# Level scores of a chunked gated attention on TensorE: four 64x64 places and one visit a level in place of two visits with copied queries

## The reference

```
f = sigmoid(f_logit)
for t in range(768):
    state = f[t][:, None] * state + outer(k[t], v[t])
    y[t] = q[t] @ state
```

## Time and profile before

| | us |
|---|---|
| median of three runs | 1084.7 |
| the profiled execution | 1084.7 |
| its span | 1082.9 |
| PE busy | 1013.7 (94%) |
| VectorE busy | 539.7 (50%) |
| ScalarE busy | 454.3 (42%) |
| GpSimd busy | 449.7 (42%) |
| chain of work that ended last: PE's share | 85% |

### The profile page before, as it was taken

One profiled execution on the slowest core, in us unless ns is written; L12 is line 12 of the kernel. 1 busy time (PEld: TensorE's weight loads), 2 busy tenths in 40 slices (PEclk: granted clock), 3 DMA queues, 4 the chain that ended last, 5 costly groups with the idle time before them and its releaser, 6 DMA issues.

```text
span 1082.9 us, 19234 instructions
## 1 busy us (share of the span) xinstructions
PE 1013.7 (94%) x7816; PEld 828.0 (76%) x7816; DVE 539.7 (50%) x743; ACT 454.3 (42%) x840; POOL 449.7 (42%) x368
## 2 busy tenths in 40 slices
PE   1484999999999999999999999999999999999997
PEld 1473778778777877877788888888888888888886
DVE  3965894885688388659736532222223222232221
ACT  6456647544753665375336532222122221222221
POOL 1856982764475366537526522212121221212121
PEclk9666999999999999999999999999999999999999
DMA  9323005202400600130043100010010010000000
GB/s 358 153 86 130 1 2 166 79 2 75 159 13 2 215 31 1 44 115 30 2 176 131 45 30 30 1 59 1 1 59 1 1 59 1 30 1 1 30 1 29
DMA packets 17367, 63.52 MB, mean 59 GB/s; under 512 B 1920, under 2 KB 2176, under 8 KB 16512
## 3 DMA queue, kind: packets, MB, share of 16 engines
q1 hardware_dynamic: 17280, 62.30, 15.9%
HBM read 52.85 MB, written 9.44 MB: 58 GB/s over the span
## 4 chain that ended last, share of the span: by engine, by line
PE 85%; issue 5%; ACT 4%; DVE 3%; POOL 2%; DMA 0%; POOLq 0%; ACTq 0%; SPq 0%; DVEq 0%
PE acc L447 11%; PE acc L448 10%; PE acc L449 10%; PE bank L474 7%; PE bank L473 7%; PE bank L475 7%; PE bank L346 6%; PE hid L433 6%; PE hid L434 5%; PE hid L435 5%; ACT scores L527 2%; PE hid L474 2%; PE hid L475 2%; PE hid L473 2%; PE bank L378 2%
## 5 line engine op out<-in xcount | busy, mean ns | idle before, releaser
L929 POOL TENSOR_TENSOR g_lo<-prod,g_hi 128x512 fp32r<-128x512 f32 x72 | 93.1, 1293 | 347.4 <-ACT g_hi L652 347.4
L922 POOL TENSOR_TENSOR g_lo<-act_tmp,g_hi 128x512 fp32r<-128x512 f32 x96 | 140.0, 1459 | 182.0 <-ACT g_hi L613 182.0
L827 DVE TENSOR_TENSOR sig<-sig,bank 128x512 f32<-128x512 f32 x72 | 49.5, 688 | 275.4 <-ACT sig L646 275.4
L740 DVE COPY_PREDICATED scores<-mask,bank 64x512 f32<-64x512 int32 x144 | 134.5, 934 | 32.7 <-PE bank L346 31.0
L652 ACT CAST g_hi<-prod 128x512 fp32r<-128x512 f32 x72 | 44.7, 621 | 247.8 <-PE acc L449 247.8
L433 PE MATMUL hid<-x_hi,win_hi 128*128 128x512 f32 x288 | 119.1, 414 | 16.1 <-DVE act_tmp L815 16.1
L882 POOL TENSOR_TENSOR keys<-keys,gates 128x512 f32<-128x512 f32 x82 | 108.0, 1317 | 57.5 <-PE bank L346 46.1
L613 ACT CAST g_hi<-act_tmp 128x512 fp32r<-128x512 f32 x96 | 59.5, 620 | 166.0 <-DVE act_tmp L815 166.0
L346 PEld LDWEIGHTS bank<-right_q,keys 128*64 128x64 f32 x2304 | 79.9, 148 | 62.4 <-issue 59.8
L346 PE MATMUL bank<-right_q,keys 128*64 128x64 f32 x2304 | 89.6, 236 | 39.6 <-ACT right_q L548 36.3
L447 PE MATMUL acc<-g_hi,wout_hi 128*128 128x512 f32 x288 | 116.9, 406 | 4.7 <-POOL g_lo L922 4.7
(11 more groups left out here) (79 smaller groups left out, 1858.7 us busy)
## 6 DMA issues: line engine op xcount, KB each, us to landing
gates<-in_f_dram SPq DMA_DIRECT2D x12, 512.0 KB, 5.4
queries<-in_q_dram SPq DMA_DIRECT2D x12, 512.0 KB, 4.9
keys<-in_k_dram SPq DMA_DIRECT2D x12, 512.0 KB, 4.8
values<-in_v_tok_dram SPq DMA_DIRECT2D x6, 1024.0 KB, 8.2
q_tok<-in_q_tok_dram SPq DMA_DIRECT2D x12, 384.0 KB, 8.1
k_tok<-in_k_tok_dram SPq DMA_DIRECT2D x12, 384.0 KB, 8.3
x_dram<-x_out SPq DMA_DIRECT2D x6, 768.0 KB, 3.2
x_raw<-x_dram SPq DMA_DIRECT2D x6, 768.0 KB, 5.5
```

Source lines behind the costliest of these rows:

```text
L740: last = dve.copy_predicated(o, level_mask(li, half), t[rows(half), :].rearrange("p (x b r) -> p x b r", x=BP, r=m))
L922: pool.tensor_tensor(g_lo[:, c % RING, :], act_tmp[:, 2 + c % 2, :], g_hi[:, c % RING, :].bitcast(F32), ALU.subtract).then_inc(g_lo_done, 1)
```

## The change

- `right_q`, its clearing and `copy_right` are gone. `level` reads the queries themselves. Each product is of one head: 64 partitions (a head's) by 64 columns of keys against 32 right queries, in the place of the array that head and half give: four places of 64x64. The two heads write into two banks.
- A level is one visit of TensorE over all 16 pairs and both heads (64 products; the last level 32), and signals `filled` by two at its end. `scale_q` and `scale_k` of both groups wait for that end.
- `take_level(a, li, e)` is by head: VectorE takes head 0 in the level's half chunk, behind the two scalings, and head 1 in the next one, for the first five levels. ScalarE takes both heads of the last two, whose entries need no mask.
- Plans are tuples: `USUAL` for units 2 to 5, with levels at half chunks (1, 4, 7, 10, 13, 16, 18); `SECOND` for unit 1, levels at (6, 9, 12, 14, 16, 18, 20), placing of the diagonal at 0, 2, 3, 4 and sigmoids at 3, 4; `FIRST` for unit 0. Unit 1 is no longer late, and its `own` and `sum_own` stand in the prologue.
- In unit 0 VectorE places the diagonals with two broadcast multiplications; ScalarE's first activation is a dummy sigmoid ahead of the data; the loads come group by group; w_in's pieces are split at every second half chunk from 4.

```diff
-H_STEP = (1, 3, 5, 7, 8, 9, 10, 12, 13, 14, 15, 17, 18, 19)
+USUAL = Plan(own=(-9, -8), diag=(-8, -7), place=(-6, -5, -4, -3), sigmoid=(-2, -1), gated=(-1, 0),
+             level=(1, 4, 7, 10, 13, 16, 18), y=(20, 20, 21, 21), y_out=(20, 21, 21, 22),
+             tk=(22, 22, 23, 23), tk_out=(23, 23, 24, 24), kv=24, decay=21, state=25, state_place=26)
+SECOND = Plan(own=(-9, -8), diag=(-8, -7), place=(0, 2, 3, 4), sigmoid=(3, 4), gated=(4, 5),
+              level=(6, 9, 12, 14, 16, 18, 20), y=(22, 22, 23, 23), y_out=(22, 23, 23, 24),
+              tk=(24, 24, 25, 25), tk_out=(25, 25, 26, 26), kv=26, decay=23, state=27, state_place=28)
+FIRST = USUAL._replace(diag=(-3, -2), sigmoid=(-3, -2), gated=(-3, -2))
...
+            for x in range(BP):
+                for half in range(2 if li < NL - 1 else 1):
+                    for e in range(2):
+                        t = slice(half * HALF, (half + 1) * HALF)
+                        if li < NL - 1:
+                            o = of(a, 2 * li + e)[rows(half), x * HALF // 2:(x + 1) * HALF // 2]
+                            q_right = queries[rows(e), x, t].rearrange("p (b s r) -> p b s r", s=2, r=m)[:, :, 1, :]
...
+                        last = pe.matmul(o, keys[rows(e), x, t], q_right, start=True, stop=True)
+            last.then_inc(filled, 2)
...
         def scale_q(a, s):
-            dve.wait_ge(q_copied, a * STEPS + s + 1)
+            dve.wait_ge(filled, fill(a, 2 * li + 2))
...
+            for li in levels_at(a, h - 1):
+                if li < NL - 2:
+                    take_level(a, li, 1)
+            for li in levels_at(a, h):
+                for g in range(2):
+                    scale_q(a, 2 * li + g)
+                if li < NL - 2:
+                    take_level(a, li, 0)
...
+        def place_diag(a, g):
+            d = diag[:, g * BP:(g + 1) * BP].rearrange("p (x a) -> p x a", a=1).broadcast_to([P, BP, P])
+            i = eye[:, :].rearrange("p (a t) -> p a t", a=1).broadcast_to([P, BP, P])
+            dve.tensor_tensor(o, i, d, ALU.mult).then_inc(diag_placed, 2)
```

More of the change, by code:

```diff
@@ L1 @@
+from collections import namedtuple
 from contextlib import ExitStack
@@ L32 @@
 PIECE = 2 * DM
+STEPS = 2 * NL
+MASKED = 2 * (NL - 2)
 Y0 = STEPS
@@ L338, in level @@
             if li:
-                pe.wait_ge(k_scaled, a * STEPS + s - 1)
+                pe.wait_ge(k_scaled, a * STEPS + 2 * li)
             else:
[L341 to L351, removed]
@@ L406, in attention @@
         def attention(a, h):
-            for s in ladder(h):
-                level(a, s)
+            for li in levels_at(a, h):
+                level(a, li)
             for b in range(B):
-                if H_Y[b] == h:
+                if PLANS[a].y[b] == h:
                     outputs(a, b)
@@ L521, in place_diag @@
                 act.wait_ge(diag_done, 2 * a + b // 2 + 1)
-            if b == 0 and a > 0:
+            if b == 0:
                 act.wait_ge(filled, fill(a - 1, TK0))
@@ L528, in place_diag, with take_level @@
             last.then_inc(diag_placed, 1)
[L530 to L539, removed]
-                if li < NL - 1:
[L541 to L545, removed]
-                else:
-                    i = i[:, :, HALF:P].rearrange("p x (s t) -> p x s t", s=2)
-                last = act.copy(o, i)
-            last.then_inc(q_copied, 1)
+        def take_level(a, li, e):
+            act.wait_ge(filled, fill(a, 2 * li + 2))
+            act.wait_ge(dve_took, a * DVE_A_UNIT + MASKED)
+            t = bank[fill(a, 2 * li + e) % 3]
+            for half in range(2):
+                if li < NL - 1:
+                    r = slice(half * HALF, half * HALF + HALF // 2)
+                    o = scores[r, :, e, (2 * half + 1) * HALF // 2:(half + 1) * HALF]
+                    last = act.copy(o, t[r, :].rearrange("p (x i) -> p x i", x=BP))
+                else:
+                    o = scores[rows(0), half::2, e, HALF:P]
+                    last = act.copy(o, t[rows(half), :].rearrange("p (x i) -> p x i", x=BP // 2))
+            last.then_inc(act_took, 1)
         def take_keys(a, b):
@@ L572, in attention @@
             for b in range(B):
-                if H_PLACE[b] == h:
+                if a > 0 and PLANS[a].place[b] == h:
                     place_diag(a, b)
             for g in range(2):
-                if H_SIGMOID[g] == h:
+                if PLANS[a].sigmoid[g] == h:
                     sigmoid(a, g)
-            for s in ladder(h + 1):
-                copy_right(a, s)
+            for li in levels_at(a, h):
+                if li >= NL - 2:
+                    for e in range(2):
+                        take_level(a, li, e)
             for b in range(B):
-                if H_Y_OUT[b] == h:
+                if PLANS[a].y_out[b] == h:
                     split_y(a, b)
@@ L723, in scale_q, with take_level @@
             dve.tensor_tensor(qr, qr, left.broadcast_to([P, BP // 2 * P // (2 * m), m]), ALU.mult).then_inc(q_scaled, 1)
[L725 to L728, removed]
+        def take_level(a, li, e):
+            dve.wait_ge(filled, fill(a, 2 * li + 2))
             if li:
[L730 to L733, removed]
+                dve.wait_ge(dve_took, a * DVE_A_UNIT + 2 * li + e - 1)
+            else:
+                dve.wait_ge(diag_placed, B * (a + 1))
+            if a == 0 and li == 0:
                 dve.wait_ge(mask_in, 16)
[L735 to L747, removed]
+            m = LEVELS[li]
+            t = bank[fill(a, 2 * li + e) % 3]
+            for half in range(2):
+                o = scores[rows(half), :, e, half * HALF:(half + 1) * HALF]
+                o = o.rearrange("p x (b s r) -> p x b s r", s=2, r=m)[:, :, :, 1, :]
+                last = dve.copy_predicated(o, level_mask(li, half),
+                                           t[rows(half), :].rearrange("p (x b r) -> p x b r", x=BP, r=m))
             last.then_inc(dve_took, 1)
@@ L873, in scale_k @@
             m = LEVELS[li]
-            pool.wait_ge(filled, fill(a, s + 1))
+            pool.wait_ge(filled, fill(a, 2 * li + 2))
             if li:
```

157 lines of the change are left out of this document (77 added, 80 removed).

## The result

The changed kernel took 1174.62 us (1172.53 to 1178.42), the kernel before 1085.23 beside it: a ratio of 1.083, 95% interval 1.080 to 1.085. The profiled execution took 1175.39 with a span of 1173.5. The forecast was 1153 (1106 to 1198). The span grew by 90.6 us.

What follows compares the result with a forecast made beforehand. TensorE was taken as the bound, busy 95.0 of 96.0 us a steady unit, behind three stretches it doesn't fill. 1084.7 + 60 (four steady units) + 7.4 (MLP unit 0) + 1 (prologue) = 1153 us, range 1106 to 1198.

Steps and rivals of the forecast that it cites:

- The wait and the queue: Steady units: activation late behind query scalings and takes on VectorE, stalls sum 18.4 us a unit.
- PE's own work: Level visits: 128 instructions at 14.6 ns, 2.22 us against 2 x 1.29, -3.4 us a unit.
- The clock: MLP units: the sum took full clock, with its fall after long stalls left to rival (b).
- rival (b): Stalls of over 4 us let the clock fall, ten costing up to 2 us each: 1173 us, 9%.
- MLP unit 0: 77.45 to 187.65 us: -8.8 at its head, level stalls 19.6, PE's work -3.4, together +7.4 us.
- The prologue: Before hidden(0): loading -6.5 us, levels 51.5 against 43.05 less about 1, net +1.
- (a): Visits: row places take turns or 14.6 ns issue is impossible; 1215 us at 29 ns, 1184 at 22 ns; 18%.
- (c): VectorE's queue has room, so the activation isn't late: -32 us, 1053 us, 11%.
- (d): Scalings never meet GpSimd: 10 - 3.4 = 6.8 us a steady unit, 1103 to 1110 us, 7%.
- (e): Gains in the head cancel the loss: no change, 2%.

Runs made afterwards that it cites:

- e9: Changed kernel, MLP work ahead of attention in the queues, VectorE's takes and GpSimd's merges later, sigmoids, gating and placings earlier: 1080.68 us, 0.9957 of the kernel before.
- e6: Changed kernel with its products reordered, all of head 0 and then all of head 1: 1243.51 us in one run.
- e7: Changed kernel where GpSimd scales only the first block of left keys from unit 1 on: 1123.27 us, ratio 1.036 to the kernel before.

## Why the prediction was right, point by point

**The wait and the queue: right, and measured to a few tenths.** Scaling pair 2.7 forecast, 2.62 measured; two takes 5.4, 5.27. The waits of a steady unit were forecast 4.75, 4.15, 2.0, 2.6, 2.0, 0.95, 0.95, measured 4.35, 3.75, 1.70, 2.11, 1.56, 0.64, 0.59. The windows (2.15 and 4.25) hold. Each wait is 0.3 to 0.5 less, for the most part because the work behind the visit is shorter than priced: from the first visit's end at 328.25 to the hidden matmul at 336.90 it is 8.65 us, where the prediction had 9.0, and behind the second 6.03 in place of 6.3. With the waits for g_lo and the gaps around visits PE stood 17 to 18 us a unit against 1.3 before (starts of MLP matmuls over 0.47 us apart, summed), so 16.3 more in the unit of the timeline.

**PE's own work: right.** Forecast 14.6 ns an instruction, measured 1.84/127 = 14.5. Where nothing waits, in levels 4 to 6 of e9's two units, five of six visits cost 2.18 to 2.20 and one 2.54, forecast 2.22, against 2 x 1.29. A unit's saving is 2.5 to 2.9 us by PE's busy time in e9, in place of 3.4. In the prologue 3.64 a visit, forecast 3.4.

**The clock: this step was mis-sized.** The sum went by full clock and left its fall to rival (b), at 9%. Behind both long waits of each steady unit the next 5 to 12 MLP matmuls ran 0.43 us apart: 336.90 to 340.73 is 3.8 us for what takes 2.05. The windows view has the granted clock (0.50 is the lower of the two levels, 1.2 GHz, 1.00 the upper, 2.4). The stretches follow the waits of 4.35, 3.75, 2.16 and 1.70 us:

```profile
336.90:340.50 3.60, 3.60 (x9) 2.79 (x9) 0.55 (x1) 2.60 (x5) 1.28 (x1) 0.53 0.20 82
348.83:354.00 5.17, 5.17 (x12) 4.12 (x13) 4.46 (x5) 2.03 (x4) 1.91 (x2) 0.50 0.00 0
257.56:262.00 4.44, 4.44 (x12) 3.51 (x13) 3.29 (x5) 1.98 (x4) 2.36 (x2) 0.62 0.00 0
363.63:365.90 2.27, 2.27 (x9) 1.61 (x9) 0.55 (x1) 1.21 (x2) 1.30 (x1) 1.00 0.00 0
```

Summed over all MLP matmuls at the low spacing, the surplus over 0.228 is 3.2 to 4.5 us a steady unit and 8.6 in MLP unit 0, 23.4 in all against 1.4 before. Which waits came before it: in the five MLP units, all of 2.60 us and more, none under 2 us when the clock had been up; of those between 2.1 and 2.4, the four at 138.36, 148.85, 159.23 and 257.56 were followed by the low level, and those at 372.41, 487.96 and 601.13 were not. A single 16.1 us wait was the only row to judge by. It was no rival but the second half of the same mechanism, and had stood in the earlier trace rows.

That 1153 + 22 of clock gives the measured 1175 is partly luck, since other errors cancel. Over the five units PE's waits grew by 12 us less than priced, and the rest of PE's time, its own work and the slower first matmuls behind waits, fell by 9 where the sum had 17. The prologue came 4 over.

**MLP unit 0: errors that partly cancel.** +13.4 against +7.4. PE's waits there grew by 7.9 (17.8 to 25.7) where 10.8 were forecast; the clock added 7.2.

**The prologue: mis-sized.** +5.3 against +1. The first visit starts at 18.98 (forecast 17.5); the chain to it runs from group 1's own product, which waited for its tokens until 12.45. Periods of the first five levels 8.9, 9.1, 7.6, 7.5 and 7.5 us, as forecast (9.1 twice, 7.6 three times). The last two were 6.9 and 5.95 in place of 5.9 and 4.6. The sixth is set by GpSimd's key scalings, for which PE waited 3.3 us; the forecast had counted the shorter query scalings. In the seventh `sum_own` for unit 1, which waited for GpSimd's own product, stands ahead of the last query scalings (68.49 and 69.36), and I had not queued it there. The visits stayed at the low level's pace (3.3/127 = 26 ns an instruction) throughout.

**Rivals.** (a) refuted by the visits and shown from the other side by e6. (c), the faster one, refuted by the timeline. (d) refuted: the scalings do meet GpSimd, 1.3 us a pair by e7; its 10 - 3.4 is 6.6 and not 6.8, under 1 us of its price. (e) refuted: the head gained 5.1 us and the rest lost 96.

The Trainium skill's "TensorE: Matmul & The Clock Gate" says in "Wait — 56ns, not 53.3ns?" that starts are never under some 25 ns apart. This case measured an average of 14.5 ns over 128 instructions in four 64x64 places, so the trace doesn't agree where places are used. It agrees with that page's "Part 3: Packing small matmuls — row/col tiling" in that tiles overlap; whether single starts lie some 4 ns apart, as it says, an average doesn't show.

## What to carry to other kernels

When a wait is moved to the end of another engine's burst, list what is queued behind it in program order, and set the time to the first instruction that the bottleneck engine needs against that engine's own work until it asks; twice the granularity (a level instead of half a level) doubled the lump and, with the new wait, broke a window with 1.9 us of slack. Put the short operations that feed the bottleneck ahead of the bulk in the queue: on VectorE alone that took back 75 of 90 us, and the same on the other queues, with later takes, another 8. And price a wait of TensorE of some 3 us or more with what follows at the low clock, here 1.2 to 2.5 us more each.

## What the runs showed of the hardware

- Four 64x64 places reach 14.5 ns an fp32 instruction at the high clock when products of the two heads (row places, each with a bank of its own) alternate, and 27.6 ns (3.50 us over 127) when one head follows the other whole, although the instructions are the same.
- VectorE's elementwise product of two SBUF operands and GpSimd's hold each other up: VectorE's pair takes 1.30 alone and 2.62 beside two key scalings, which themselves take 3.97 there and 2 x 1.53 by the earlier trace rows.
- In the changed kernel's prologue the clock column says 1.00 from 18.95 to 72.37 us, while the matmul spacing (26 ns in place of 14.5) and the weight loads (223 ns in place of 135, rows below) are slower by 1.8 and 1.65, and a matmul's time went from 219 to 291 ns, as it went from 222 to 314 before, where the column read 0.65. I read it as the low level; in short bursts the spacing is the better witness.

A visit of the changed kernel in a steady unit, and below it one in its prologue, by the view of one line (shortest, median and longest in ns, and the stretch):

```profile
L353 PEld LDWEIGHTS bank<-queries,keys x128: 129/135/135, 326.2 to 328.0; 64*64 64x64 f32 x128
```
```profile
L353 PEld LDWEIGHTS bank<-queries,keys x128: 175/223/228, 36.9 to 40.2; 64*64 64x64 f32 x128
L353 PE MATMUL bank<-queries,keys x128: 280/291/313, 36.9 to 40.3; 64*64 64x32 f32 x128
```
